# Moving the low parts of x and the rings of g to other offsets in SBUF, in a gated linear attention with two dense blocks

## What is computed

```python
# attention, f = sigmoid(f_logit)
state = f[:, :, t, :, None] * state + k_t outer v_t
y[:, :, t] = q_t @ state
# first block
h = x @ w_in                       # (3072,384) @ (384,2048)
g = where(h >= 1, h, where(h <= -1, 0, (h + 1) ** 2 / 4))
x = g @ w_out                      # (3072,2048) @ (2048,384)
# second block
g = (a0 + a1*h + a2*h*h + a3*h*h*h) / (1 + |b0|*|h| + |b1|*h*h + 1e-6)
out = g @ w_out
```

## Time and profile before

| | |
|---|---|
| three runs | 958.5, 961.0, 961.23 us |
| profiled execution | 958.65 us, its span 956.8 us |
| mean granted TensorE clock | 0.99 |
| TensorE busy | 914.6 us (96%), 4626 matmuls |
| VectorE, ScalarE, GpSimd busy | 77%, 60%, 29% |
| time of all DMA packets | 17% of 16 engines' span |

### The profile page before, as it was taken

One profiled execution on the slowest core, in us unless ns is written; L12 is line 12 of the kernel. 1 busy time (PEld: TensorE's weight loads), 2 busy tenths in 40 slices (PEclk: granted clock), 3 DMA queues, 4 the chain that ended last, 5 costly groups with the idle time before them and its releaser, 6 DMA issues.

```text
span 956.8 us, 12944 instructions
## 1 busy us (share of the span) xinstructions
PE 914.6 (96%) x4626; PEld 744.0 (78%) x4626; DVE 737.0 (77%) x909; ACT 571.4 (60%) x725; POOL 277.8 (29%) x202
## 2 busy tenths in 40 slices
PE   4789999999999999999999989999999999999996
PEld 3668778888888888888888867788888888888884
DVE  7977786776677666777556499998888888888883
ACT  5545435434443444443355588788788787887872
POOL 3454410000000100000046555335234343353223
PEclk9989999999999999999999989999999999999999
DMA  6434312111211211230123320010010010010000
GB/s 187 119 81 122 114 34 83 34 57 60 66 34 34 83 35 34 71 87 1 34 83 91 91 66 1 1 66 0 0 66 0 0 66 0 33 33 0 33 1 36
DMA packets 27510, 48.68 MB, mean 51 GB/s; under 512 B 5312, under 2 KB 8384, under 8 KB 27456
## 3 DMA queue, kind: packets, MB, share of 16 engines
q1 hardware_dynamic: 27456, 48.00, 17.0%
HBM read 36.18 MB, written 9.44 MB: 48 GB/s over the span
## 4 chain that ended last, share of the span: by engine, by line
PE 78%; DVE 12%; issue 4%; ACT 3%; POOL 1%; POOLq 0%; DMA 0%; SPq 0%; DVEq 0%; ACTq 0%
PE acc L1076 18%; PE h_pair L1060 18%; PE acc L1120 18%; PE at_pair L1098 9%; PE h_pair L1098 9%; DVE growth L791 2%; PE at_pair L1002 2%; PE at_pair L1021 2%; PE at_pair L1016 1%; PE at_bank L1030 1%; DVE t L860 1%; DVE s L886 1%; DVE t L895 1%; DVE s L891 1%; POOL g_lo L513 1%
## 5 line engine op out<-in xcount | busy, mean ns | idle before, releaser
L513 POOL TENSOR_TENSOR g_lo<-g,g_hi 128x1024 fp32r<-128x1024 f32 x48 | 116.9, 2436 | 231.8 <-DVE t L895 227.3
L622 ACT CAST g_hi<-g 128x512 fp32r<-128x512 f32 x96 | 59.6, 621 | 170.5 <-DVE g L867 170.5
L860 DVE SCALAR_TENSOR_TENSOR t<-t 128x512 f32<-128x512 f32 x96 | 74.2, 773 | 90.0 <-ACT t L615 89.4
L615 ACT ACTIVATE t<-h_pair,half 128x512 f32<-128x512 f32 x96 | 65.9, 686 | 100.8 <-PE h_pair L1060 100.1
L1060 PE MATMUL h_pair<-x_hi,w_hi 128*128 128x512 f32 x288 | 113.5, 394 | 4.9 <-DVE x_lo L855 4.9
L1076 PE MATMUL acc<-g_hi,w_hi 128*128 128x512 f32 x288 | 118.2, 410 | 0.0
L471 POOL TENSOR_TENSOR k_s<-k_in,growth 128x512 f32<-128x512 f32 x22 | 30.6, 1389 | 298.3 <-DVE growth L791 297.5
L1120 PE MATMUL acc<-g_hi,w_hi 128*128 128x512 f32 x288 | 113.9, 395 | 1.5 <-POOL g_lo L513 1.4
L1076 PE MATMUL acc<-g_lo,w_hi 128*128 128x512 f32 x288 | 114.3, 397 | 0.0
L1076 PE MATMUL acc<-g_hi,w_lo 128*128 128x512 f32 x288 | 114.2, 396 | 0.0
L1120 PE MATMUL acc<-g_hi,w_lo 128*128 128x512 f32 x288 | 113.6, 394 | 0.0
(11 more groups left out here) (136 smaller groups left out, 2028.0 us busy)
## 6 DMA issues: line engine op xcount, KB each, us to landing
w_raw<-w SPq DMA_DIRECT2D x32, 384.0 KB, 3.3
f_in<-fC SPq DMA_DIRECT2D x48, 96.0 KB, 2.9
k_in<-kC SPq DMA_DIRECT2D x48, 96.0 KB, 2.4
q_in<-qC SPq DMA_DIRECT2D x48, 96.0 KB, 2.3
mlp_out<-o_sb SPq DMA_DIRECT2D x18, 256.0 KB, 3.2
x_raw<-mlp_out SPq DMA_DIRECT2D x6, 768.0 KB, 4.4
outT<-o_sb SPq DMA_DIRECT2D x18, 256.0 KB, 2.0
v_in<-vC SPq DMA_DIRECT2D x22, 192.0 KB, 2.6
```

The lines of the kernel that those rows point to most:

```text
L513: nc.gpsimd.tensor_tensor(g2_lo[r][:, :, :], g2[r][:, :, :], g2_hi[r][:, :, :].bitcast(F32), ALU.subtract).then_inc(lo2_ready, 1)
L615: nc.scalar.activation(t1[n % 2][:, :], h1[n % 2], ACT.Relu, scale=0.5, bias=half[:, :]).then_inc(relu1_ready, 1)
L622: nc.scalar.copy(g1_hi[n % R1][:, :], g1[n % 2][:, :]).then_inc(hi1_ready, 1)
L860: nc.vector.scalar_tensor_tensor(out=t1[n % 2][:, :], in0=t1[n % 2][:, :], scalar=1.0, in1=t1[n % 2][:, :], op0=ALU.min, op1=ALU.mult).the ...
```

## The change

Three places get extra bytes ahead of them. No instruction, wait or size changes, and each engine's instructions and waits stand in the same order as before. The number of places of the g2 ring below `ring_at` is the same too.

```diff
@@ -43,6 +43,7 @@
 LAG2 = 4
 R2 = 4
+G2_SHIFTS = [0, 0, 0, 0, 32, 64, 64, 64]
 HEAD = 4
@@ -108,6 +109,7 @@
         x_hi = lay.tile("x_hi", [P, KT, 2 * NB], F32R)
+        lay.at += 32
         x_lo = lay.tile("x_lo", [P, KT, 2 * NB], F32R)
@@ -161,7 +163,9 @@
         for r in range(R2):
+            lay.at += G2_SHIFTS[2 * r]
             g2_hi.append(lay.tile(f"g2_hi{r}", [P, UW, NB], F32R))
+            lay.at += G2_SHIFTS[2 * r + 1]
             g2_lo.append(lay.tile(f"g2_lo{r}", [P, UW, NB], F32R))
```

## The result

The changed kernel takes 962.88 us (median of 16 runs, 961.8 to 964.39) against 959.41 us for the kernel before (16 runs). The ratio is 1.0038, with a 95% interval of 1.0031 to 1.0045: 3.5 us slower, where 2.8 us faster was forecast. The time lies inside the stated range, which ran from 948 us to over 967, on the wrong side of no change.

A forecast was written before the change was run, and what follows sets the result against it. TensorE, busy without a gap in both dense blocks, was taken as the bound, through matmul spacing. Terms -3.6, +1.6, -0.8 and 0 summed to -2.8 us, from the median 961.0 to 958.2 us; range 948 to over 967.

The forecast's parts named there:

- All of it lies on the path: Both dense blocks: the whole summed gain of -2.8 us shortens the time, since TensorE sets the pace there.
- The half clock as a sign that places matter: Matmuls of x and g: equal spacing at half clock, so the 14 and 20 ns extra at full clock fit colliding reads.
- For +32 the mirror image: Matmuls reading x_lo, moved from 0 to +32: 230.5 ns spacing, 576 x +2.8 = +1.6 us.
- the slower rival: x_lo and most g matmuls: starts at odd multiples of 32 bytes cost more, +6.0 us, 967.0 us; chance 0.26.
- alternating them loses it for x_hi too: Groups of x: if their even spacing needs x_hi and x_lo at one offset, x_hi slows too; no size in the sum.
- For -32 the middle of its two known neighbours: g in the first block and ring places 0 and 1: 230.5 ns spacing, 1296 x -2.8 = -3.6 us.
- the terms for places 2 and 3: g2 ring, second block: g2_hi2 at 0 gains 0.8 us; g2_lo2 (+64), g2_hi3 (+128) and g2_lo3 (+192) change nothing.
- Places don't matter: Dense blocks: the spacing step between x and g may come from PSUM banks, so no change, 961.0 us; chance 0.18.
- Low multiples bad: x_lo and most g matmuls: odd multiples of 32 bytes make streams touch an extra 64-byte piece, 967.0 us; chance 0.26.
- its own sign: Second block chain: g groups at places 0 and 1 over 4.20 us and x groups over 4.15 would prove this rival.
- A clean place: g at -32 and three far offsets: some offset avoids collision, half of 20 ns goes, 944 us; chance 0.14.
- The argument against that rival: Weights take 512 bytes while the matmul passes 2048 in little more than one load, so reads meet at any offset.

The follow-up runs named there:

- all at 0: Kernel before, with all high and low parts of g1 and g2 moved to the weights' place modulo 512 bytes, where x already lay: 948.83 us against 959.49, ratio 0.9885.

## Why the prediction was wrong

**What bounds the kernel: right, but for one stretch.** TensorE is busy throughout, and the spacing sets the time. The first eight steps of the second block are different. From the first product of x of that block to the 145th takes 63.1 us before (535.9 to 599.0), 63.0 after and 63.0 with all at 0. Its window before, where TensorE waits and VectorE has 52 of 61 us:
```profile
536.00:597.00 61.00, 56.22 (x234) 44.95 (x233) 51.99 (x41) 50.85 (x53) 29.91 (x21) 0.94 0.15 46
```
"All of it lies on the path" was too wide by the 234 products of 3456 in that stretch (144 of x, 72 of g, and 18 of g that end the first block). That would have changed the forecast by 0.2 us.

**The half clock as a sign that places matter: right.** The version with all of g at 0 shows it, where places alone moved g from 233 to 227 ns. The rule of the Trainium skill that I set against it ("TensorE: Matmul & The Clock Gate", "Step-by-step: what each phase is for": two independent read ports, so a load takes nothing from a running matmul) leaves no room for a price of the distance. These runs show one: the same matmul beside the same load takes 226.8 or 234.1 ns, by the distance of the two tiles. Even the best place is 13 ns over the 213.5 of 512 columns.

**The step that failed first: "For +32 the mirror image, also 230.5 ns, as nothing in the rows prefers a sign: 576 x +2.8 = +1.6 us".** Both factors were wrong. The price of 32 bytes is not half of that of 64; it is the full one, 233.5 ns for g, and 232.8 for x with both its parts there. And the count is not the 576 matmuls that read x_lo but all 1728 of x, since the neighbours pay. Measured: +5.4 us in the changed kernel. I had named this under the slower rival ("alternating them loses it for x_hi too") and left it out of the sum.

**The second: "For -32 the middle of its two known neighbours, 230.5 ns", and with it "1296 x -2.8 = -3.6 us".** Measured with x_lo in its old place, g gains 0: 233.3 and 233.4 ns against 233.2 and 233.4. Two points of a curve were taken for a slope. These two terms, off by 3.8 and 3.6 us, are more than the whole miss of 6.3 us in the median; the terms for places 2 and 3 came to -0.8 us forecast and -0.9 measured (216 x -1.9 + 216 x -2.1). That agreement is luck: the forecast had all of it from g2_hi2 and nothing from place 3, and the trace has half of it from each place, with g2_hi2 at 231 to 232 ns and not at x's 227.8.

**The rivals.** "Places don't matter" fell with the version at 0. "Low multiples bad", whose 967.0 us had the right sign, fell as a cause. Offsets that are multiples of 64 or 128 bytes cost as much (232.8 at 128, 233.3 at 192), and moving everything by 64 changes nothing. By its own sign, too, g at places 0 and 1 should have gone over 4.20 us, and the groups of g in the chain went to 4.16 to 4.19. "A clean place" put half of the 20 ns on some new offset. None of them has that; the best place is 0, where x lay already, and it keeps 13 ns. The change moved x_lo off it and put most of g on other dear places. The argument against that rival, that the two reads must meet once at any offset, is not settled by this.

**What stays open** is which reads collide. The experiments show that the distance between weights and moving operand modulo 256 decides, and that one displaced tile slows the matmuls around it. They speak against a stream colliding only with the load beside it, and against one colliding only with its own weights. That a collision of reads is the mechanism at all is argued from the distances; no run shows it directly. I have no mechanism that gives all the spacings.

## What to carry to other kernels

Where TensorE is busy without a gap, take the spacing of its matmuls by moving operand: two kinds of the same size with different spacings say that something other than their size sets it, and the places in SBUF are a candidate that costs nothing to change. Here the weights and every moving operand at the same place modulo 256 bytes gave 1.15%, and a single tile in the stream off that place gave nearly all of it back. And two points of an unknown curve are not a slope; where a forecast hangs on the third point, keep both ends and look whether neighbours share the price.

## What the runs showed that I had not expected

- The period is 256 bytes, with one best place (226.8 ns), one half-good (+64, 229.7) and the rest at 232.8 to 234.1.
- A displaced operand slows matmuls whose own operands are in place: g at 0 stood at 231.1 ns in the first block when only x_lo was off, and at 228.1 when nothing was.
- The version with all of g at 0 gives less than its spacings say. x gains 2.5 and 1.0 ns and g 5.1 and 6.6, 864 times each, 13.1 us, but the time falls by 10.7 and the profiled span by 5.3. About 0.7 us of the 13.1 lie in the 63 us that never got shorter. And in its profiled execution, the longest of its five, the granted clock fell at two more places, at 112 to 124 and 596 to 606 us, where it was 1.00 before. This is the first, before and in this version:
```profile
112.00:124.00 12.00, 12.00 (x82) 10.01 (x82) 8.83 (x14) 6.05 (x11) 6.93 (x7) 1.00 0.26 78
112.00:124.00 12.00, 10.29 (x45) 8.41 (x46) 9.31 (x16) 5.61 (x9) 5.18 (x7) 0.72 0.36 98
```
TensorE waited 2.5 us for VectorE just before (to 113.7 us, [2.53 <-DVE state L860] in the timeline), and from 117.3 to 119.5 us its matmuls of 512 columns are 0.43 us apart, as at the half clock. The version moved by 64 bytes, with the same spacings, kept 1.00 at 596 to 606 us and has a span of 947.6 us; at 112 to 124 us its clock fell as well (0.73).
